# The second batch's first down projection in the rounded f32 format, from split operands

## The reference, cut to what matters

```python
def _moe_ref(x, U, V, w_ch1, w_ch2):
    xt = x.transpose(0, 2, 1)
    h = xt @ U @ V
    u = x + h.transpose(0, 2, 1)
    ch = np.maximum(u @ w_ch1, 0.0) @ w_ch2
    return (u + ch).astype(np.float32)
```

## Time and profile before

| | us |
|---|---|
| median of three runs | 651.81 (651.49 to 652.59) |
| the profiled execution | 651.69 |
| its span in the trace | 649.9 |
| PE busy, share of the span | 632.0, 97% |
| DVE, ACT, POOL busy | 329.9, 317.8, 366.6 |
| granted TensorE clock | 1.0 of full speed |

### The profile page before, as it was taken

The page is one execution under the profiler, slowest core; times in us unless marked ns, Lnnn a source line. Parts: engine busy times, 40 slices in busy tenths (PEclk is TensorE's granted clock), DMA queues, the critical chain, the costliest instruction groups (busy, mean ns, idle before and its releaser), DMA issues.

```text
span 649.9 us, 10391 instructions
## 1 busy us (share of the span) xinstructions
PE 632.0 (97%) x3554; PEld 567.2 (87%) x3554; DVE 329.9 (51%) x718; ACT 317.8 (49%) x723; POOL 366.6 (56%) x373
## 2 busy tenths in 40 slices
PE   8999999999999999999999999999999999999997
PEld 7889788988989987989999988899998888899986
DVE  7776543343333422567576652286668225675411
ACT  5667555454454452645445444455444455444321
POOL 8545456555556474365756563575756544757262
PEclk9999999999999999999999999999999999999999
DMA  7434253443325234223233333243233343431142
GB/s 174 112 78 129 64 134 91 122 114 95 84 82 162 82 88 123 68 78 114 75 104 82 113 95 102 82 113 105 74 114 97 98 141 87 150 91 38 49 141 86
DMA packets 88420, 65.51 MB, mean 101 GB/s; under 512 B 43024, under 2 KB 72464, under 8 KB 88368
## 3 DMA queue, kind: packets, MB, share of 16 engines
q1 hardware_dynamic: 88368, 64.85, 35.5%
HBM read 61.42 MB, written 3.15 MB: 99 GB/s over the span
## 4 chain that ended last, share of the span: by engine, by line
PE 87%; DVE 4%; ACT 3%; POOL 3%; issue 2%; DMA 1%; DVEq 0%; ACTq 0%; SPq 0%; POOLq 0%
PE bank L1378 33%; PE bank L1172 21%; PE bank L1344 10%; PE bank L1234 4%; PE bank L1207 4%; PE bank L1215 3%; PE bank L1308 3%; PE bank L1271 3%; PE bank L1252 2%; POOL w_lo L759 1%; PE bank L1192 1%; PE bank L1285 1%; ACT w_hi L780 1%; PE bank L1370 1%; DVE masked L966 1%
## 5 line engine op out<-in xcount | busy, mean ns | idle before, releaser
L759 POOL TENSOR_TENSOR w_lo<-w_raw,w_hi 128x512 fp32r<-128x512 f32 (+1 forms) x158 | 205.7, 1307 | 167.5 <-ACT w_hi L780 167.2
L780 ACT ACTIVATE w_hi<-w_raw 128x512 fp32r<-128x512 f32 (+1 forms) x158 | 96.2, 617 | 57.9 <-PE bank L1378 39.2
L1172 PE MATMUL bank<-b_hi,a_hi 128*128 128x384 f32 x280 | 94.6, 338 | 1.0 <-DVE temps L1078 0.6
L1172 PE MATMUL bank<-b_lo,a_hi 128*128 128x384 f32 x280 | 94.8, 339 | 0.0
L1378 PE MATMUL bank<-w_hi,hid_hi 128*128 128x512 f32 x216 | 87.8, 406 | 0.6 <-POOL w_lo L759 0.6
L1378 PE MATMUL bank<-w_hi,hid_lo 128*128 128x512 f32 x216 | 85.1, 394 | 0.0
L1378 PE MATMUL bank<-w_lo,hid_hi 128*128 128x512 f32 x216 | 84.7, 392 | 0.0
L812 ACT ACTIVATE probs<-masked,neg_max 128x264 f32<-128x264 f32 x96 | 49.5, 516 | 66.3 <-DVE neg_max L966 65.8
L1378 PE MATMUL bank<-w_hi,y_hid 128*128 128x512 f32 x216 | 71.0, 394 | 0.2
L966 DVE CUSTOM_DVE_ANT_0 masked<-bank,masks 128x264 f32<-128x264 f32 x96 | 41.1, 430 | 48.5 <-PE bank L1207 44.9
L724 POOL COPY p_sink<-probs 128x12 f32<-128x12 f32 x96 | 19.3, 203 | 71.9 <-ACT probs L812 70.4
(11 more groups left out here) (142 smaller groups left out, 1409.6 us busy)
## 6 DMA issues: line engine op xcount, KB each, us to landing
w_raw<-in_moe_w_ch_dram SPq DMA_DIRECT2D x144, 256.0 KB, 2.7
w_raw<-in_moe_w_ch_dram SPq DMA_DIRECT2D x20, 512.0 KB, 3.5
q_nat<-in_q_dram SPq DMA_DIRECT2D x12, 256.0 KB, 3.0
k_nat<-in_k_dram SPq DMA_DIRECT2D x12, 256.0 KB, 3.7
v_nat<-in_v_dram SPq DMA_DIRECT2D x12, 256.0 KB, 3.6
out_dram<-o_stage SPq DMA_DIRECT2D x11, 256.0 KB, 3.4
w_raw<-in_moe_w_tok_dram SPq DMA_DIRECT2D x6, 256.0 KB, 2.7
w_raw<-in_moe_w_tok_dram SPq DMA_DIRECT2D x8, 192.0 KB, 2.3
```

The costliest lines, as they stand in the source:

```text
L759: nc.gpsimd.tensor_tensor(w_lo[:, split % NW, 0:n], w_raw[:, split % NR, 0:n], w_hi[:, split % NW, 0:n].bitcast(f32), ALU.subtract) \
L780: nc.scalar.activation(w_hi[:, split % NW, 0:n], w_raw[:, split % NR, 0:n], ACT.Copy) \
L1172: last = mm(bank[:, 0:HALF], w[at % 2][:, a, k, :], u[:, b_part, k, :], start=(first and n == 0), stop=(n == 5), skip_group_check=True)
```

## The change

For batch 1 alone, the down projection works on rounded parts. U's stationary block has 128 columns: U high three times, U low once (`U4_parts`, in free columns behind the x2 slots). x is split into high and low by ACT and DVE in the two x2 slots. Each step is two matmuls in place of one plain f32 matmul, with x high and with x low. The result has four groups of 32 rows; the fourth, U low times x, meets a fourth copy of V (V high) in the products with V, which run over 128 rows for batch 1 and over 96 for batch 0 still.

New steps: `usplit` (two ACT copies, of 384 and 192 columns, two DVE subtractions, of 128 and 64), `x1split` t for six t (one ACT copy and one DVE subtraction of 128 x 512 each). x1split 2 to 5 wait on ACT until the down step two before is done (`down1_done`), and each down step waits on PE for `x1_split`. The units of the preparation become ten: usplit with x1split 0 and 1 stands where the first downs stood (behind mm1 10), and all that follows comes one place later: downs behind mm2 9 (with x1split 2, 3), mm1 11 (with x1split 4, 5) and mm2 10, ups behind mm1 12, mm2 11, mm1 13 and mm2 12, T splits behind mm1 14 and mm2 13. wload 0, 1, 2, wsum 0, 1 and wsplit 0 are counted from the end and come one place later as well.

```diff
--- before.py
+++ after.py
@@ -142,7 +142,9 @@
         if layer == 1:
-            units = [[("down", 1, b, 2 * c), ("down", 1, b, 2 * c + 1)] for c in range(NQ // 2)]
+            split = [[("x1split", 2 * c), ("x1split", 2 * c + 1)] for c in range(NQ // 2)] + [[]]
+            units = [[("usplit",)] + split[0]]
+            units += [[("down", 1, b, 2 * c), ("down", 1, b, 2 * c + 1)] + split[c + 1] for c in range(NQ // 2)]
         else:
@@ -289,8 +291,8 @@
         U3_sb = sb("U3_sb", [P, NQ, 3 * RANK])
-        V3_sb = sb("V3_sb", [3 * RANK, S], f32r)
-        low3 = sb("low3", [3 * RANK, DM], f32r)
+        V4_sb = sb("V4_sb", [4 * RANK, S], f32r)
+        low4 = sb("low4", [4 * RANK, DM], f32r)
         with ExitStack() as before_u:
@@ -308,7 +310,7 @@
         sink_raw = o_stage[0:3 * HS, 0:B, :]
-        V3_raw = o_stage[0:3 * RANK, :, :].rearrange("p a b -> p (a b)")[:, 0:S]
+        V4_raw = o_stage[0:4 * RANK, :, :].rearrange("p a b -> p (a b)")[:, 0:S]
 
@@ -339,6 +341,8 @@
                         for part in (b_hi, b_lo))
+        U4_parts = [part[:, 5:7].rearrange("p a k t -> p (a k t)")[:, 2 * DM:2 * DM + n * P]
+                    .rearrange("p (t r) -> p t r", t=n) for part, n in ((b_hi, KD), (b_lo, NQ - KD))]
         with ExitStack() as before_y:
...
@@ -654,8 +663,8 @@
                     sp.wait_ge(vsink_split, B)
-                    for n in range(3):
-                        sp.dma_start(V3_raw[n * RANK:(n + 1) * RANK, :], moe_V).then_inc(V_loaded, 16)
+                    for n in range(4):
+                        sp.dma_start(V4_raw[n * RANK:(n + 1) * RANK, :], moe_V).then_inc(V_loaded, 16)
                 elif s[0] == "pv" and s[1] == (NQ - 2) * H + 4:
@@ -829,7 +838,18 @@
                 elif s[0] == "down" and s[1] == 1 and s[3] == NQ - 1:
-                    high_of((s[:3], 0), 3 * RANK, low3[:, :], ACT.Copy)
+                    rows = (4 if s[2] else 3) * RANK
+                    high_of((s[:3], 0), rows, low4[0:rows, :], ACT.Copy)
+                elif s[0] == "usplit":
+                    act.wait_ge(x_ready, NTILES)
+                    for part, ts in zip(U4_parts, (slice(0, KD), slice(KD, NQ))):
+                        nc.scalar.activation(part[:, :, 0:3 * RANK], U3_sb[:, ts, :], ACT.Copy).then_inc(u_high, 1)
+                elif s[0] == "x1split":
+                    t = s[1]
+                    act.wait_ge(x_ready, NTILES)
+                    if t >= 2:
+                        act.wait_ge(down1_done, t - 1)
+                    nc.scalar.activation(x2_hi[:, t % 2, :], x_nat[:, 1, t, :], ACT.Copy).then_inc(x1_high, 1)
                 elif s[0] == "down" and s[1] == 2 and s[3] == NQ // 2 - 1:
@@ -993,15 +1013,26 @@
                     if T == 2:
-                        dve.wait_ge(V_loaded, 48)
-                        nc.vector.tensor_copy(V3_sb[:, :], V3_raw).then_inc(V_high, 1)
+                        dve.wait_ge(V_loaded, 64)
+                        nc.vector.tensor_copy(V4_sb[:, :], V4_raw).then_inc(V_high, 1)
                         dve.wait_ge(V_high, 1)
-                        part = V3_sb[2 * RANK:3 * RANK, :]
-                        nc.vector.tensor_tensor(part, V3_raw[2 * RANK:3 * RANK, :], part.bitcast(f32),
+                        part = V4_sb[2 * RANK:3 * RANK, :]
+                        nc.vector.tensor_tensor(part, V4_raw[2 * RANK:3 * RANK, :], part.bitcast(f32),
                                                 ALU.subtract).then_inc(V_split, 1)
...
                     rows = slice(RANK, 2 * RANK)
-                    low_of((s[:3], 0), rows, low3[rows, :], low3[rows, :])
+                    low_of((s[:3], 0), rows, low4[rows, :], low4[rows, :])
+                elif s[0] == "usplit":
+                    dve.wait_ge(U_loaded, 48)
+                    for n, (part, ts) in enumerate(zip(U4_parts, (slice(0, KD), slice(KD, NQ)))):
+                        dve.wait_ge(u_high, n + 1)
+                        nc.vector.tensor_tensor(part[:, :, 3 * RANK:4 * RANK], U3_sb[:, ts, 0:RANK],
+                                                part[:, :, 0:RANK].bitcast(f32), ALU.subtract).then_inc(u_split, 1)
+                elif s[0] == "x1split":
+                    t = s[1]
+                    dve.wait_ge(x1_high, t + 1)
+                    nc.vector.tensor_tensor(x2_lo[:, t % 2, :], x_nat[:, 1, t, :], x2_hi[:, t % 2, :].bitcast(f32),
+                                            ALU.subtract).then_inc(x1_split, 1)
                 elif s[0] == "down" and s[1] == 2 and s[3] == NQ // 2 - 1:
@@ -1248,9 +1279,19 @@
                         m_free(use)
-                    pe.wait_ge(x_ready, NTILES if b else t + 1)
-                    last = mm(m_tile(use)[0:3 * RANK, :], U3_sb[:, t, :], x_nat[:, b, t, :],
-                              start=(t == 0), stop=(t == NQ - 1), skip_group_check=True)
+                    if b:
+                        pe.wait_ge(u_split, 2)
+                        pe.wait_ge(x1_split, t + 1)
+                        for n, x in enumerate((x2_hi, x2_lo)):
+                            last = mm(m_tile(use)[:, :], U4_parts[t // KD][:, t % KD, :], x[:, t % 2, :],
+                                      start=(t == 0 and n == 0), stop=(t == NQ - 1 and n == 1),
+                                      skip_group_check=True)
+                        if t < NQ - 1:
+                            last.then_inc(down1_done, 1)
+                    else:
+                        pe.wait_ge(x_ready, t + 1)
+                        last = mm(m_tile(use)[0:3 * RANK, :], U3_sb[:, t, :], x_nat[:, b, t, :],
+                                  start=(t == 0), stop=(t == NQ - 1), skip_group_check=True)
                     if t == NQ - 1:
@@ -1298,7 +1339,8 @@
                         if layer == 1:
-                            last = mm(m_tile((s[:4], d))[:, 0:HALF], low3[:, rows], V3_sb[:, cols],
+                            ranks = slice(0, (4 if b else 3) * RANK)
+                            last = mm(m_tile((s[:4], d))[:, 0:HALF], low4[ranks, rows], V4_sb[ranks, cols],
                                       start=False, stop=True, skip_group_check=True)
@@ -1363,7 +1405,8 @@
                             if layer == 1:
-                                mm(m_tile(use)[:, :], V3_sb[:, here], low3[:, :], start=True, stop=False,
+                                ranks = slice(0, (4 if b else 3) * RANK)
+                                mm(m_tile(use)[:, :], V4_sb[ranks, here], low4[ranks, :], start=True, stop=False,
                                    skip_group_check=True)
```

More of the change, by code:

```diff
@@ L396, in attention_then_two_mixers @@
         tp_ready = sem("tp_ready")
+        u_high = sem("u_high")
+        u_split = sem("u_split")
+        x1_high = sem("x1_high")
+        x1_split = sem("x1_split")
+        down1_done = sem("down1_done")
         q_copied = sem("q_copied")
```

## The result

| | before | after |
|---|---|---|
| median | 651.72 (651.39 to 652.73, 22 runs) | 653.08 (651.43 to 655.23, 22 runs) |
| profiled execution, its span | 651.69, 649.9 | 652.93, 651.1 |

A forecast was written before the change was run, and what follows sets the result against it. PE was taken to bound the kernel (87% of the span). Its 2.39 us gain, less a 0.84 wait, is eaten by the T-split tail; mm2 15 starts 0.31 later, so +0.3 gives 652.1 us, range 650.2 to 653.3.

The forecast's parts named there:

- PE's own gain, 2.39: Layer 1 down projection on PE: twelve rounded matmuls take 2.77 us where the plain f32 ones took 5.16.
- X: PE's wait at the first pair of down steps for x 0 and x 1, 0.84 us.
- Second and third pair at nothing: Later down steps: x 2 to x 5 are split before PE needs them, slack 0.4 to 0.5 us, cost 0.
- Rival 3: DVE between 254 and 259: x's low parts meet POOL's w_lo at each pair, +1.7 us, 653.8 us; chance 0.10.
- T3 late by POOL: Preparation's end on DVE: T3's subtraction alternates with POOL's w_lo of chunk 63, takes about 2.0 us, ends at 280.1.
- Rival 1: T splits on DVE: T3 goes ahead of POOL, mm2 15 begins at 282.3, -0.74 us, 651.1 us; chance 0.26.
- mm2 15 at 283.37, PE there at 280.72, idle 2.6: End of preparation: last mm2 waits for hid_lo 15 behind the T splits and starts 0.31 us later than before.
- rival 2: Tail before mm2 15: T splits don't hold hid_hi 15 back, PE's gain shows, -2.3 us, 649.5 us; chance 0.12.
- Moved steps in attention, p_sink, V at nothing: Attention: later weight loads, sums, splits and the fourth V copy cost 0; p_sink 0 to 0.3 us, taken as 0.
- Rival 4: Down projection: matmuls on these views stay as slow as before (5.16 us), ups 2.4 later, 654.5 us; chance 0.02.
- mm1 10 ending at 250 as before: Ahead of the first down steps on PE: the end of mm1 10 stays at 250 us, an expected sign.

The follow-up runs named there:

- two kernels with T3 and T4 moved: T3 and T4 splits put behind mm1 15: in the changed kernel 648.99 us (0.9962), in the kernel before 650.53 us (0.9982).
- the experiment with the empty unit: Changed kernel with usplit and x1split 0, 1 in the empty place ahead of mm1 10, no later step moved: 650.59 us (0.9983).
- kernel with the shift alone: Kernel before, plain f32 downs, one more empty unit ahead of the preparation: 653.48 us, in another batch 654.72 us.

## Why the forecast was right in its steps and 1 us low

Times of after are given less 1.07, the shift that was there at mm1 10's end.

- **PE's own gain, 2.39.** Right: three groups of 0.91 to 0.92, and 2.5 between two kernels that differ in this alone apart from the place of the splits and of the second weights' sums.
- **X = 0.84.** Right: 0.89. It came as one wait (0.67 from start to start, 0.51 of it idle) and a wider spacing (0.30 for 0.23) in place of two waits. The 1.58 between the two kernels with T3 and T4 moved says the same.
- **Second and third pair at nothing.** Right, no idle. Rival 3 falls for this kernel; the experiment with the empty unit shows that its mechanism is real (1.18 us of waits) where DVE is late.
- **T3 late by POOL, about 2 us.** Right: the three splits end at 281.00, less 1.07 is 279.93; 280.1 predicted. Taking POOL away from them gave 1.04 back. Rival 1 (DVE keeps the port) falls. The row from the next mixer was read too narrowly: the two subtractions that took 4.02 met two POOL subtractions, one that had begun at 425.67 besides the one at 427.13, so each meeting cost 1.03. The sum used one meeting at that price, and it holds. The Trainium skill (SBUF - State Buffer, SBUF: two separate sides), which I had cited, lets only one engine at a time have the shared ports. This trace agrees: T3's subtraction takes some 2.0 for 0.95 while POOL's takes 1.87 for 1.29. Who is next is what the runs add: here the waiting POOL step got in between two DVE steps that were queued back to back.
- **mm2 15 at 283.37, PE there at 280.72, idle 2.6.** Right: 283.31, 280.69 (281.53 + 0.23 - 1.07) and 2.46. The gain of 1.55 in front was lost in the tail, as rival 2 would not have it. The kernel with the shift alone shows how large the loss was: it stood at 34.90 for 33.08, +1.82 with nothing gained.
- **Moved steps in attention, p_sink, V at nothing.** V measured, nothing. The rest is not tried by itself; from mm1 10's end back the profile shows no difference but the program's start.
- **Rival 4 (as slow as before).** Falls by the first point.
- **The sign "mm1 10 ending at 250 as before".** Missed by 1.07 in the first profile, met in the second (249.75): it belongs to the program's start.

**What failed** is no step of the order but a term that stands in none of them. "It stands for 2.6 us" was costed as 2.6 us of standing, covered by PE's gain in front, and the work behind it at its old speed ("behind it PE runs on the seven products without a break, and the rest shifts with it"). I had a granted clock of 1.0 in one profiled execution and took it for a constant. In most executions (26 of 34) the mean clock was low, and in the one of these that was profiled it was half speed behind this idle, +1.6 us. Some of the 26 fell elsewhere, as 19 of 66 do in the kernel before; by the times it was here in about nine of the twelve later ones. With PE kept busy in the gap the kernel takes 651.47, as the kernel before does; the difference to 653.06 is 1.6. Forecast +0.3, order +0.25; and counted from the 651.3 to 651.4 of its later executions at full clock, the clock's +1.6 gives 652.9 to 653.0, the median but for 0.1. In the first 22 executions late starts, like that of the profiled one, have an unknown part in it. That the time still lay in the range is in part luck: the range was made for other terms, and no term in it was the clock.

**What stays open:** what beside its length decides whether the clock falls behind such an idle (the same 2.46 in the shifted kernel: mean clock low in 1 of 6 executions on one chip, 4 of 5 on another; 1.78: 3 of 11, no more than the kernel before has). The changed kernel was not run on those two chips beside its variants, so how much of this is the chip is not shown. Also why the program's start varies by 1 us between executions, and whether the change has a part in it; and what lowers the clock between 70 and 100 us in about a quarter of them, with or without the change.

## What to carry to other kernels

Work saved on the leading engine is paid out only if what it waits for next also comes sooner: here 1.55 us of net gain ran into a tail of splits that the new unit had moved 1.82 back, and putting hid_lo 15 ahead of two of them brought 0.8 us from the mark to mm2 15 without the change and 2.6 with it (1.1 and 4.1 in the medians, the second with the clock in it). An idle on TensorE has two prices, its length and the clock behind it, and the second one can be the larger. One profiled execution doesn't show the second: look at the mean clock of all timed executions, and if they fall into groups, get a trace from each.

## What the runs showed of the hardware that I had not expected

- An idle of 2.46 us on TensorE was followed by half speed for some 3 us in two of the four profiled executions that had one (after, the changed kernel again, and the shifted kernel twice), 1.5 to 1.6 us of loss. The fall began some 0.7 us after PE had resumed in the one case (clock 0.97 from 280 to 284, matmuls 0.23 apart at first, 0.43 from 283.81) and about when it resumed in the other (the first matmul took 0.77).
- 18 transposes of 128 x 128 took 2.13 us in that gap, some 0.12 each, and brought 1.6 us against the changed kernel of another batch: cheap filler, where the gap can't be closed.
- Two engines at the shared port: three DVE subtractions of 128 x 768 took 3.79 for 2.75 with one POOL subtraction of 128 x 512 among them, and that one 1.87 for 1.29. Both sides pay; what DVE loses (1.04) is less than POOL's undisturbed 1.29.
